# Experts' first product in two fp16 parts, over x that is reloaded, scaled and split into slots

## The reference

```
P = exp(x @ w_gate - max);  8 times: rows, then columns of P normalized
for e in range(8):                       # w1[e]: 320 x 1024, w2[e]: 1024 x 320
    out += P[:, e:e+1] * (maximum(x @ w1[e], 0) @ w2[e])
then  elu(out @ w_in) @ w_out            # 320 x 2048, 2048 x 320
```

## Time and profile before

| | us |
|---|---|
| median of 3 runs (2073.25 to 2074.62) | 2073.81 |
| the profiled execution's own time | 2073.23 |
| its span, first to last instruction | 2071.4 |
| mean granted TensorE clock | 0.998 |
| busy: PE, DVE, ACT, POOL | 2052.2, 1368.2, 957.6, 532.1 |

### The profile page before, as it was taken

The page is one execution under the profiler, slowest core; times in us unless marked ns, Lnnn a source line. Parts: engine busy times, 40 slices in busy tenths (PEclk is TensorE's granted clock), DMA queues, the critical chain, the costliest instruction groups (busy, mean ns, idle before and its releaser), DMA issues.

```text
span 2071.4 us, 37327 instructions
## 1 busy us (share of the span) xinstructions
PE 2052.2 (99%) x14954; PEld 1639.3 (79%) x14954; DVE 1368.2 (66%) x2590; ACT 957.6 (46%) x1818; POOL 532.1 (26%) x523
## 2 busy tenths in 40 slices
PE   9999999999989999999999999999999999999999
PEld 8999998888967777777777777777777778999998
DVE  7888887654667665666666666666666566666665
ACT  6877777432334434434434444344344344333333
POOL 7878777211322102111011011021021111010100
PEclk9999999999999999999999999999999999999999
DMA  7454453311110000000000000000100000000001
GB/s 122 73 82 74 72 81 63 100 31 49 41 41 10 20 29 1 28 29 1 29 29 1 29 29 1 29 18 12 29 1 29 29 1 16 1 28 29 1 26 51
DMA packets 193408, 70.61 MB, mean 34 GB/s; under 512 B 153040, under 2 KB 189392, under 8 KB 193232
## 3 DMA queue, kind: packets, MB, share of 16 engines
q1 hardware_dynamic: 193232, 68.19, 14.9%
HBM read 60.31 MB, written 7.86 MB: 33 GB/s over the span
## 4 chain that ended last, share of the span: by engine, by line
PE 96%; DVE 2%; POOL 1%; DMA 0%; ACT 0%; issue 0%; SPq 0%; DVEq 0%
PE up L1621 20%; PE up L1580 13%; PE yps L1680 9%; PE yps L1682 9%; PE yps L1681 9%; PE up L1628 7%; PE yps L1597 4%; PE yps L1596 4%; PE yps L1595 4%; PE yps L1300 3%; PE up L1315 2%; PE up L1265 2%; PE up L1300 1%; PE yps L1347 1%; PE misc L1347 1%; PE up L1323 1%
## 5 line engine op out<-in xcount | busy, mean ns | idle before, releaser
L1680 PE MATMUL yps<-w2h_top,hh_top 128*128 128x320 f16 x1344 | 406.1, 302 | 4.9 <-DVE hh_rest L2133 4.8
L1681 PE MATMUL yps<-w2h_rest,hh_top 128*128 128x320 f16 x1344 | 402.6, 300 | 0.0
L1682 PE MATMUL yps<-w2h_top,hh_rest 128*128 128x320 f16 x1344 | 402.6, 300 | 0.0
L2148 DVE SCALAR_TENSOR_TENSOR tok<-yps,share,tok 128x320 f32<-128x320 f32 x672 | 337.8, 545 | 91.3 <-PE yps L1682 88.2
L1003 ACT ACTIVATE up<-up 128x512 f32<-128x512 f32 x252 | 146.7, 582 | 367.0 <-PE up L1621 359.7
L1680 PEld LDWEIGHTS yps<-w2h_top,hh_top 128*128 128x128 f16 x1344 | 131.0, 97 | 134.7 <-issue 69.3
L770 POOL TENSOR_TENSOR w1l<-w1l_raw,w1h 128x768 fp32r<-128x768 f32 x68 | 101.4, 1492 | 524.9 <-ACT w1h L896 523.5
L2133 DVE SCALAR_TENSOR_TENSOR hh_rest<-hl_raw,hh_top 128x512 f16<-128x512 f32 x168 | 117.5, 700 | 146.7 <-ACT hh_top L1015 146.7
L2133 DVE SCALAR_TENSOR_TENSOR hh_rest<-up,hh_top 128x512 f16<-128x512 f32 x168 | 115.5, 687 | 134.5 <-ACT hh_top L1015 134.4
L1597 PE MATMUL yps<-w2h,hl 128*128 128x320 f32 x576 | 177.8, 309 | 0.0
L1596 PE MATMUL yps<-w2l,hh 128*128 128x320 f32 x576 | 177.5, 308 | 0.0
(11 more groups left out here) (280 smaller groups left out, 4469.1 us busy)
## 6 DMA issues: line engine op xcount, KB each, us to landing
w2l_raw<-in_moe_w SPq DMA_DIRECT2D x16, 640.0 KB, 5.5
w1l_raw<-in_moe_w SPq DMA_DIRECT2D x32, 256.0 KB, 3.1
xr_raw<-x_dram SPq DMA_DIRECT2D x12, 512.0 KB, 4.1
w1l_raw<-in_moe_w SPq DMA_DIRECT2D x32, 128.0 KB, 3.6
wp<-in_w SPq DMA_DIRECT2D x24, 160.0 KB, 3.2
rp<-in_r SPq DMA_DIRECT2D x24, 160.0 KB, 3.3
vp<-in_v SPq DMA_DIRECT2D x24, 160.0 KB, 3.6
raw<-in_a SPq DMA_DIRECT2D x24, 160.0 KB, 3.6
```

Of the source, the lines that this page charges most:

```text
L1680: nc.tensor.matmul(o, h_top[:, tile, c], wh, start=first, stop=False)
L1681: nc.tensor.matmul(o, h_top[:, tile, c], wl, start=False, stop=False)
L1682: ins = nc.tensor.matmul(o, h_rest[:, tile, c], wh, start=False, stop=last)
L2148: nc.vector.scalar_tensor_tensor(out=acc, in0=yps[:, s, 0:DM], scalar=share[:, buf, blk * NSUB + s:blk * NSUB + s + 1], in1=acc, op0=ALU.m ...
```

## The change

The first product of the fast groups takes its operands as two fp16 parts too. The weights' parts lie in the place of the fp32r ones (`w1_halves`). The token tiles are written a second time: SP reloads all of x in pairs (three tiles a block, 1.5 MB a pair in place of 1 MB), ScalarE multiplies it by a factor from x's greatest value (`scale_x`), GpSimd makes the four combinations into tiles of their own (`mixes`), and ScalarE and GpSimd split nine tiles a pair in place of four (`pair_hi`, `pair_lo`). The fp16 parts lie in slots over the fp32r x, so a slot is free only when group 1 has used what lies there (`slot_free`). The greatest of x becomes a reduction of its own on GpSimd at the end of group 0. Since the rest of the weights no longer lies over their raw form, SP loads the weights of group g when those of g-2 are split, one group earlier for the first product's. `most_down` of group 3 moves from set 0 to set 1 of group 2, and `scale_up(2)` and the first splits of group 2 come earlier in group 1. The counts and sizes of the matmuls stay.

```diff
+        def with_slots(name, rows, blocks):
+            slots = ExitStack()
+            made = slots.enter_context(nc.sbuf_tensor(f"{name}_slots", [P, rows, blocks, 2, TB], F16))
+            slots.close()
...
+        xh, x_slots = ([made] for made in with_slots("xh0", 2, 1))
+        xl, mix_slots = ([made] for made in with_slots("xl0", 2, 1))
+        xt, tail_slots = ([made] for made in with_slots("xt0", 1, 1))
...
+        mixes = sb("mixes", [P, NB, TB])
...
+        def slot_of(tiles, t, blk):
+            at = tiles[0][:, t, 0] if blk == 0 else tiles[1][:, t, blk - 1]
...
+            return [slot_of(mix_slots, i % 2, 2 * j + i // 2) for i in range(4)]
...
+        def pair_tiles(j):
+            first, second = 2 * j, 2 * j + 1
+            t1, t2, t3, t4 = ((mixes[:, i, :], *mixed(j)[i]) for i in range(4))
+            return [(xr[:, 0, 0, :], *slot_of(x_slots, 0, first)), (xr[:, 0, 1, :], *slot_of(x_slots, 1, first)),
+                    (xr[:, 0, 2, :], tail16(first), None), t1, t2,
+                    (xr[:, 1, 1, :], *slot_of(x_slots, 1, second)), (xr[:, 1, 2, :], tail16(second), None), t3, t4]
+        PAIR_TILES = 9
+        def slot_free(j, i):
+            return STEPS + NF * (2 * j + (1 if i < 5 else 2))
...
-                tiles = [raw_w2[g % 2], *w2_halves[g % 2]]
+            if is_fast(g):
+                tiles = [w[g % 2] for w in ((raw_w2, w2_halves) if kind == "down" else (raw_w1, w1_halves))]
...
-            load_mixed(0)
+            load_pair(0)
             sp.wait_ge(s_down, STEPS * NSUB)
             group_weights(sp, 2)
             for j in range(1, TPAIRS):
-                sp.wait_ge(s_mixlo, 4 * j)
-                load_mixed(j)
+                sp.wait_ge(s_mixlo, PAIR_TILES * j)
+                load_pair(j)
             sp.wait_ge(s_down, 2 * STEPS * NSUB)
...
                 if is_fast(g - 2):
                     sp.wait_ge(s_wlo, split_tasks(g - 1))
-                    down_weights(sp, g)
-                    sp.wait_ge(s_fdown, (g - 1 - FIRST_FAST) * SETS * 2 * NSUB)
-                    up_weights(sp, g)
                 else:
                     sp.wait_ge(s_down, (plain_no(g - 2) + 1) * STEPS * NSUB)
-                    group_weights(sp, g)
...
+                pool.wait_ge(s_xscaled, 2 * (j + 1))
+                b11, b21, b12, b22 = (xr[:, q, t, :] for q in range(2) for t in range(2))
+                t1, t2, t3, t4 = (mixes[:, i, :] for i in range(4))
+                link(nc.gpsimd.tensor_tensor(t1, b12, b11, ALU.subtract))
+                link(nc.gpsimd.tensor_tensor(t2, b22, t1, ALU.subtract))
+                nc.gpsimd.tensor_tensor(t3, b22, b12, ALU.subtract)
+                nc.gpsimd.tensor_tensor(t4, b21, t2, ALU.subtract).then_inc(s_mixsum, 1)
...
+            def pair_lo(j, some=range(PAIR_TILES)):
                 for i in some:
-                    pool.wait_ge(s_mixhi, 4 * j + i + 1)
-                    hi, lo = mixed(j)[i]
-                    nc.gpsimd.tensor_tensor(lo, raw_mixed[i], hi.bitcast(F32), ALU.subtract).then_inc(s_mixlo, 1)
+                    pool.wait_ge(s_mixhi, PAIR_TILES * j + i + 1)
+                    raw, hi, lo = pair_tiles(j)[i]
+                    if i in (2, 3, 6, 7):
+                        pool.wait_ge(s_mixlo, PAIR_TILES * j + i)
+                    if lo is None:
+                        raw, hi, lo = (tile[TAIL:P] for tile in (raw, hi, hi))
+                    nc.gpsimd.tensor_tensor(lo, raw, hi, ALU.subtract).then_inc(s_mixlo, 1)
...
-            mix_tokens(0)
+            pool.wait_ge(s_xmost, 1)
+            nc.gpsimd.partition_all_reduce(x_top_all[:], x_top[:], P, RMAX).then_inc(s_xall, 1)
             pool.wait_ge(s_lmax, 1)
             nc.gpsimd.partition_all_reduce(gmax[:], lmax[:], P, RMAX).then_inc(s_gmax, 1)
-            mixed_lo(0)
+            mix_tokens(0)
+            pair_lo(0)
             most_of(2)
-            mix_tokens(1)
-            mixed_lo(1, range(0, 2))
             mix_weights(2)
             split_lo(2, range(0, 2))
-            mixed_lo(1, range(2, 4))
+            mix_tokens(1)
+            pair_lo(1)
             split_lo(2, range(2, len(FAST)))
             mix_tokens(2)
-            mixed_lo(2, range(0, 2))
+            pair_lo(2, range(0, 4))
             most_of(3)
-            mixed_lo(2, range(2, 4))
+            pair_lo(2, range(4, PAIR_TILES))
             mix_weights(3)
             all_split(3)
...
+                if t == 0 and is_fast(g - 2):
+                    act.wait_ge(s_fdown, (g - 1 - FIRST_FAST) * SETS * 2 * NSUB)
...
+            def scale_x(j, q):
+                act.wait_ge(s_xfactor, 1)
+                act.wait_ge(s_mixraw, (j + 1) * 2 * 3 * 16)
+                nc.scalar.activation(xr[:, q, :, :], xr[:, q, :, :], ACT.Copy, scale=x_factor[:, 0:1])\
+                  .then_inc(s_xscaled, 1)
+            def pair_hi(j, *some):
+                for i in some:
+                    act.wait_ge(s_up, slot_free(j, i))
+                    act.wait_ge(s_xscaled, 2 * j + (1 if i < 3 else 2))
+                    if i in (3, 4, 7, 8):
+                        act.wait_ge(s_mixsum, j + 1)
+                    raw, hi, _ = pair_tiles(j)[i]
+                    nc.scalar.activation(hi, raw, ACT.Copy).then_inc(s_mixhi, 1)
...
-                if 5 <= k < 9:
-                    mixed_hi(0, k - 5)
+                if k in (2, 3):
+                    scale_x(0, k - 2)
+                for j, first in ((0, 5), (1, 16)):
+                    at = (first, first + 1, first + 3, first + 4) if j == 0 else range(first, first + 4)
+                    if k in at:
+                        pair_hi(j, *((0, 1, 2), (3, 4), (5, 6), (7, 8))[at.index(k)])
+                if k == 11:
+                    scale_up(2)
                 if k == 12:
-                    scale_up(2)
-                if k == 13:
                     scale_down(2)
-                if k in (14, 15, 18, 19):
-                    mixed_hi(1, (14, 15, 18, 19).index(k))
-                if k in (16, 17, 20, 21, 22, 23):
-                    split_hi(2, (16, 17, 20, 21, 22, 23).index(k))
+                if k in (13, 14, 20, 21, 22, 23):
+                    split_hi(2, (13, 14, 20, 21, 22, 23).index(k))
+                if k in (13, 14):
+                    scale_x(1, k - 13)
+                if k in (22, 23):
+                    scale_x(2, k - 22)
...
-                wh, wl = (w[buf][:, i, left, :] for w in (w1h, w1l))
+                wh, wl = (w[:, i, left, :] for w in w1_halves[buf])
...
+                if g == FIRST_FAST and fp == 0:
+                    pe.wait_ge(s_mixlo, PAIR_TILES * (j + 1))
...
-                if soon and n == 0:
+                if soon and n == (1 if g == FIRST_FAST else 0):
                     most_down(soon)
...
                 dve.wait_ge(s_mostall, g - FIRST_FAST + 1)
-                nc.vector.tensor_scalar(unit[:, 0:1], most_all[:, 3:4], TINY, DM / HALF_MOST, ALU.max, ALU.mult)
                 nc.vector.tensor_scalar(inverse_of[:, 1:2], most_all[:, 2:3], TINY, 1.0 / HALF_MOST, ALU.max, ALU.mult)
-                link(nc.vector.scalar_tensor_tensor(out=unit[:, 1:2], in0=most_all[:, 0:1], scalar=TINY,
+                link(nc.vector.scalar_tensor_tensor(out=unit[:], in0=most_all[:, 0:1], scalar=TINY,
                                                     in1=most_all[:, 1:2], op0=ALU.max, op1=ALU.max))
-                link(nc.vector.tensor_tensor(inverse_of[:, 0:1], unit[:, 0:1], unit[:, 1:2], ALU.mult))
+                link(nc.vector.tensor_scalar(inverse_of[:, 0:1], unit[:], 1.0 / UP_MOST, None, ALU.mult))
                 nc.vector.reciprocal(factor[:], inverse_of[:]).then_inc(s_factor, 1)
                 link(nc.vector.tensor_tensor(back[:], inverse_of[:, 0:1], inverse_of[:, 1:2], ALU.mult))
+                link(nc.vector.tensor_tensor(back[:], back[:], x_inverse[:], ALU.mult))
+            def x_scale():
+                dve.wait_ge(s_xall, 1)
+                link(nc.vector.tensor_scalar(x_inverse[:], x_top_all[:], TINY, 1.0 / UP_MOST, ALU.max, ALU.mult))
+                nc.vector.reciprocal(x_factor[:], x_inverse[:]).then_inc(s_xfactor, 1)
```

More of the change, by code:

```diff
@@ L260, in build @@
         tok = sb("tok", [P, NT, DM])
[L261 removed]
+        for made, to in zip(with_halves("w1h1", [P, FPAIRS, 9, P]), (w1h, w1_halves)):
+            to.append(made)
         low_weights(1)
@@ L264, in build @@
             to.append(made)
[L265 to L270 removed]
+        for name, rows, *to in (("xh1", 2, xh, x_slots), ("xl1", 2, xl, mix_slots), ("xt1", 1, xt, tail_slots)):
+            for made, kept in zip(with_slots(name, rows, NB - 1), to):
+                kept.append(made)
+        mixes = sb("mixes", [P, NB, TB])
+        lrow = mixes.rearrange("p t n -> p (t n)")[0:E]
         seventh = sb("seventh", [P, TB])
@@ L274, in build @@
         x_most = sb("x_most", [P, 2 * NB])
-        most = sb("most", [P, 4])
-        most_all = sb("most_all", [P, 4])
-        unit = sb("unit", [P, 2])
```

(30 more changed lines are left out.)

73 lines of the change are left out of this document (23 added, 50 removed).

## The result

The changed kernel takes 2038.96 us (median of 4 runs, 2038.73 to 2039.33), the kernel before 2074.18 us beside it (4 runs, 2073.25 to 2074.62): ratio 0.983, 95% interval 0.981 to 0.985. It is 35 us faster where 46 us were forecast; the time lies inside the range. The profiled execution has a span of 2037.3 us against 2071.4.

A forecast was written before the change was run, and what follows sets the result against it. TensorE, busy 99% of the span, was taken to bound the kernel. Terms -45 - 6.5 + 1.4 + 1.5 + 1.9 + 0.4 = -46.3 gave 2026.9, or 2027.5 us at the runs' median; range 2018 to 2042.

The forecast's parts named there:

- The price of a matmul: TensorE, fast groups' first product: an fp16 matmul of 512 columns costs 0.2156 us, where fp32r costs 0.2286.
- rivals 2 and 3: 2: fp16 gains nothing at 512 columns, no change (0.04). 3: fp16's 512 columns cost no more than 320, 1833 us (0.01).
- The set, -45 us: 84 fast sets: each falls from 13.40 to 12.86 us by cheaper first-product matmuls, the copy's wait staying at 0.10.
- up to 0.1 us a set: Fast sets: given back if some copy or rest had only just been in time, 8 us; kept for the range.
- waits in the later groups: Listed sign in the profile after that the forecast is wrong; no size given.
- The transfer, -6.5 and +1.4: Group 2: moving the reduction saves the first fast set's wait and half clock, -6.5 us; VectorE late in set 1, +1.4.
- Group 1, +3.8: TensorE waits in group 1: step 12's `hi` +1.5 us, step 14's `hi` and rest +1.9; VectorE's slower small operations +0.4.
- +0.4: VectorE's small operations are slower while GpSimd works: +0.4 us.
- Later pairs at nothing: Later pairs of x meet slack, the third pair's larger transfer included: no cost, 2 us kept for the range.
- Rival 1: Group 1's set-up work holds TensorE longer: two more waits of 4.3 us with half clock, +13, 2040 us; chance 0.17.
- Rival 4: The clock falls at group 1's end and stays low; with ten sets at that level 2155 us; chance 0.05.
- PEclk under 0.9 in a fast group: Listed sign in the profile after that the forecast is wrong: TensorE's granted clock below 0.9 in a fast group.

The follow-up runs named there:

- type alone: The kernel before, with the fast groups' first product read from one constant fp16 tile: 2036.25 us, ratio 0.982.
- split wait: The changed kernel with VectorE's first take ahead of its fourth rest, and TensorE waiting for that rest only before the matmuls that read it: 2029.26 us, ratio 0.979.
- set-up alone: The changed kernel, with the fast groups' first product read from one constant fp32r tile: 2073.05 us, ratio 1.000.

## Why the prediction was right, and where it was wrong

- **The price of a matmul**, 0.2156 us, was right within 1 ns (0.216); rivals 2 and 3 are out. This is what made the forecast right: the gain is TensorE's, by the price of its matmuls, and the type alone gave it.
- **The set, -45 us** is the step that failed in size: 0.455 us a set, 38 us. The copy's wait fell to 0.03 us instead of staying at 0.10, and VectorE's take added 0.13. (The forecast's 6.51 for 48 x 0.136 is 6.53; that is the other 0.02 of the 12.94.) The sentence that VectorE's idle time keeps a shorter set off the path was wrong: it argued from a busy share (66%), where the chain from TensorE's tail product over VectorE's sum, ScalarE's copy and two rests to the take had no slack. The forecast had kept "up to 0.1 us a set" for the range; it belonged in the sum, and its own sign of being wrong, "waits in the later groups", came. The type alone and the split wait show it.
- **The transfer, -6.5 and +1.4**: wait and half clock of the first set went, and the second set's wait was 1.73. That is over the bound of 1.5, which counted only the moved reduction: with the same lists at the old type (set-up alone) it was 1.38 us, so the rest comes from the shorter products ahead of it. Missing was the third set's 2.95 us and the clock behind it. Together the three sets gave 2.5 us and not the 6.7 of the forecast (with the shorter products in it).
- **Group 1, +3.8**: the two forecast waits came, 1.65 for +1.5 and 0.97 for +1.9. The two of 1.47 and 1.45 us were in the term "+0.4" for VectorE's slower operations. This was too small by a factor of seven: it had no working behind it, and the cause is the same as in the third set. The wait in step 11 varies (1.1 us in other runs), so some 0.5 us of group 1's excess over the forecast belongs to this execution alone.
- **Later pairs at nothing** was right as to the transfer: ScalarE is idle for only 0.2 us ahead of the third pair's scaling.
- **Rival 1** had the right kind of event (two more waits), without its half clock in group 1. **Rival 4**: the clock fell again, to 0.65 in one window of 4 us, and came back. The forecast's "near 1.00 all through" was wrong there, and "PEclk under 0.9 in a fast group", a sign of being wrong, came in this window.

In sum: 6 us from the sets behind the third, 4 from the first three, 2 from group 1 make up the 12 us that were missing. Since errors of terms with one sign added up, the result came out near the range's far end. It lies inside because the range reached up to rival 1's 2040; the size of the new waits as a whole was not foreseen.

## What to carry to other kernels

When the bounding engine gets faster, take the chain through the other engines that returns to it, and write down its slack in hundredths of a us at each wait; an average busy share doesn't tell. An elementwise instruction of VectorE on SBUF alone (not a reduction or a reciprocal) is priced by what GpSimd does at that moment, so place or cut GpSimd's long instructions away from VectorE's short, linked ones. Where one queue is reordered, list what every instruction behind it gates, transfers among them.
